# Moving the wait for a slot-table scatter from GpSimd to the load queue, the scatters behind the eighth sum, and an x2 copy ahead of a relu

## The reference

```python
for t in range(S):                        # attention, per batch and head: B, H, S, D = 4, 8, 768, 40
    m_new = np.maximum(f_gate[:, :, t] + m, i_gate[:, :, t])
    f_stab, i_stab = np.exp(f_gate[:, :, t] + m - m_new), np.exp(i_gate[:, :, t] - m_new)
    C = f_stab * C + i_stab * np.einsum('bhd,bhe->bhde', vt, kt)
    n = f_stab * n + i_stab * kt
    y[:, :, t] = sigmoid(o) * einsum(C, qt) / max(|n . qt|, 1)
x = y as (3072 tokens, 320)
h = x @ w_in                              # 320 x 2048
g = where(h >= 1, h, where(h <= -1, 0, (h + 1) ** 2 / 4))
x = g @ w_out                             # 2048 x 320
logits = x @ w_gate                       # 8 experts, the largest takes the token
out[mask] = gate_w * (relu(x[mask] @ w1[e]) @ w2[e])
```

## Time and profile before

| what | us |
|---|---|
| median of three runs | 878.41 (877.98 to 883.18) |
| the profiled execution, its own time | 891.37 |
| its span, first to last instruction | 889.5 |
| TensorE busy in the span | 792.6 (89%) |
| VectorE, ScalarE, GpSimd busy | 581.5, 407.9, 446.9 |
| mean granted TensorE clock, as a share of full speed | 0.958 |

### The profile page before, as it was taken

The page is one execution under the profiler, slowest core; times in us unless marked ns, Lnnn a source line. Parts: engine busy times, 40 slices in busy tenths (PEclk is TensorE's granted clock), DMA queues, the critical chain, the costliest instruction groups (busy, mean ns, idle before and its releaser), DMA issues.

```text
span 889.5 us, 17627 instructions
## 1 busy us (share of the span) xinstructions
PE 792.6 (89%) x5858; PEld 770.5 (87%) x5858; DVE 581.5 (65%) x965; ACT 407.9 (46%) x689; POOL 446.9 (50%) x357
## 2 busy tenths in 40 slices
PE   1799999899999999999899999806998999998975
PEld 1788999899989999999899999705998999998964
DVE  5565878597778877786878783445545666655440
ACT  2024454344444444453444444415656667666451
POOL 3352534344434434443443533326878887877742
PEclk9999999899999999999999999957999999999988
DMA  6931222424342332324222300040485313366730
GB/s 189 306 121 66 67 81 80 66 67 89 66 100 48 128 51 93 65 80 65 80 65 80 80 0 16 16 139 23 137 263 160 104 39 102 111 197 195 243 130 4
DMA packets 46887, 89.20 MB, mean 100 GB/s; under 512 B 6421, under 2 KB 29273, under 8 KB 46850
## 3 DMA queue, kind: packets, MB, share of 16 engines
q1 hardware_dynamic: 42962, 79.63, 32.4%
q0 software_dynamic: 3888, 9.08, 3.2%
HBM read 103.56 MB, written 9.33 MB: 127 GB/s over the span
## 4 chain that ended last, share of the span: by engine, by line
PE 54%; DMA 14%; issue 9%; DVE 8%; POOL 8%; ACT 4%; SPq 1%; POOLq 0%; DVEq 0%; ACTq 0%
PE bank L1270 14%; PE bank L1258 14%; DMA raw<-in_w 6%; PE bank L1449 6%; PE bank L1396 5%; DMA slot_table<-pair,dsti 4%; POOL w_tl L465 4%; PE bank L1214 3%; PE bank L1205 2%; PE bank L1230 2%; PE bank L1221 2%; POOL g_t L509 1%; PE bank L1411 1%; DVE g_l L951 1%; DMA tab<-slot_table,rowi 1%
## 5 line engine op out<-in xcount | busy, mean ns | idle before, releaser
L509 POOL TENSOR_TENSOR g_t<-u_t,r_t 128x512 f32<-128x512 f32 x96 | 132.3, 1378 | 216.6 <-ACT u_t L657 202.8
L652 ACT ACTIVATE r_t<-bank,neg 128x512 f32<-128x512 f32 x96 | 65.9, 686 | 220.2 <-PE bank L1258 195.9
L1270 PE MATMUL bank<-wo_h,g_h 128*128 128x328 f32 x384 | 130.1, 339 | 10.7 <-ACT x2s L669 8.7
L1270 PE MATMUL bank<-wo_h,g_l 128*128 128x328 f32 x384 | 122.8, 320 | 0.0
L1270 PE MATMUL bank<-wo_l,g_h 128*128 128x328 f32 x384 | 122.3, 319 | 0.0
L945 DVE TENSOR_SCALAR u_t<-bank 128x512 f32<-128x512 f32 x96 | 65.7, 685 | 78.1 <-ACT r_t L652 54.0
L1059 DVE TENSOR_TENSOR w_l<-raw,w_h 128x1024 fp32r<-128x1024 f32 x38 | 64.5, 1701 | 46.7 <-ACT w_th L723 46.5
L465 POOL TENSOR_TENSOR w_tl<-raw,w_th 128x512 fp32r<-128x512 f32 x38 | 72.5, 1931 | 30.9 <-ACT w_th L723 30.8
L1270 PEld LDWEIGHTS bank<-wo_h,g_h 128*128 128x128 f32 x384 | 74.5, 194 | 15.1 <-ACT x2s L669 10.1
L657 ACT ACTIVATE u_t<-u_t,half 128x512 f32<-128x512 f32 x96 | 69.4, 723 | 38.4 <-DVE u_t L945 38.4
L1258 PE MATMUL bank<-xT_h,wi_h 128*128 (+1 forms) x384 | 78.6, 287 | 1.6 <-issue 1.6
(11 more groups left out here) (210 smaller groups left out, 2084.0 us busy)
## 6 DMA issues: line engine op xcount, KB each, us to landing
raw<-in_w SPq DMA_DIRECT2D x19, 1280.0 KB
raw<-in_w SPq DMA_DIRECT2D x19, 1024.0 KB
W<-decays SPq DMA_DIRECT2D x24, 512.0 KB, 5.2
raw<-in_w SPq DMA_DIRECT2D x38, 256.0 KB
kS<-in_ktok SPq DMA_DIRECT2D x24, 256.0 KB
qT<-in_qt SPq DMA_DIRECT2D x48, 80.0 KB
kT<-in_kt SPq DMA_DIRECT2D x48, 80.0 KB
vS<-in_v SPq DMA_DIRECT2D x24, 160.0 KB, 5.1
```

The lines of the kernel that those rows point to most:

```text
L509: pool.tensor_tensor(g_t[p % 2][:, :], u_t[p % 2][:, :], r_t[p % 2][:, :], ALU.add).then_inc(sm["g_done"], 1)
L652: act.activation(r_t[p % 2][:, :], bank_h[p % 2][:, :], ACT.Relu, bias=neg1[:, 0:1]).then_inc(sm["r_done"], 1)
L1270: mm = pe.matmul(bank_acc[tt][:, 0:DL], l[p % 4][:, c], r[:, f, :], start=f == 0 and a == 0, stop=f == NT1 - 1 and a == 2)
```

## The change

The wait of `table_free` moves from GpSimd's program to the load queue's, behind `store_x2(t-1)`, with the first release of `pair`. GpSimd's `to_table` moves behind the sum of p = 7, and its waits for the last scatters stand ahead of the table's gather. ScalarE's `x2_copy` moves ahead of `relu_part(t, 2)`.

```diff
@@ block.sync
             for tt in range(2):
                 sp.sem_inc(x2_st[tt], 16)
+            sp.sem_inc(sm["pair_free"], 1)
@@ block.sync, behind store_x2
+            def table_free(t):
+
+                for tt in range(2):
+                    sp.wait_ge(slots_st[tt], (t + 1) * 16)
+                sp.sem_inc(sm["pair_free"], 1)
+
@@ block.sync, body
                 if prev:
                     store_x2(t - 1)
+                    table_free(t - 1)
@@ block.gpsimd
-            pool.sem_inc(sm["pair_free"], 1)
@@
-            def table_free(t):
-
-                for tt in range(2):
-                    pool.wait_ge(slots_st[tt], (t + 1) * 16)
-                pool.sem_inc(sm["pair_free"], 1)
-
@@ block.gpsimd, body and tail
-                    if prev and p == 7:
-                        to_table(t - 1)
                     gated(t, p)
                 if prev:
-                    table_free(t - 1)
+                    to_table(t - 1)
 
             def tail(t):
                 to_table(t)
-                table_free(t)
@@ block.gpsimd, behind all_blocks
+            for tt in range(2):
+                pool.wait_ge(slots_st[tt], 16 * NBLK)
             pool.wait_ge(sm["row_ready"], 1)
@@ block.scalar, body
                         x_high(t + 1, 0)
+                    if prev and p == 2:
+                        x2_copy(t - 1, 0)
+                        x2_copy(t - 1, 1)
                     relu_part(t, p)
@@
-                    if prev and p == 2:
-                        x2_copy(t - 1, 0)
-                        x2_copy(t - 1, 1)
                     square_part(t, p)
```

## The result

The changed kernel takes 983.34 us in the median of four runs (982.53 to 987.84), the kernel before 878.19 in the same session: a ratio of 1.117, 95% interval 1.112 to 1.121. That is 105.2 us more. The prediction was 975.0 us, with 948 to 1008 as its range. The profiled execution of the changed kernel took 982.53 us with a span of 980.7, so between the two profiled spans lie 91.2 us.

What follows compares the result with a forecast made beforehand. TensorE was taken to bound the stage. Nine bodies 11.1 us longer each add 99.6 us, the last block takes off 3.0, so 96.6 us on the median of 878.41 gives 975.0 us; range 948 to 1008.

Steps and rivals of the forecast that it cites:

- The mechanism: Load queue: next body's loads stand behind the wait for late scatters, so TensorE stalls ahead of L1205, nine times.
- The chain of the forecast: Block end at 406 us: last `first`, sum, scatters, landing, SP, kS load, then `scores`; a stall of 10.9 us.
- Half clock: TensorE returns from each stall at the lower clock level, 1.2 GHz, losing 1.7 us a block.
- The 3.3 us: Work TensorE does at half clock behind a stall, read from two earlier stretches; half of it is lost.
- the 40.83: TensorE's own work in one block, from the period 366.86 to 407.69 without idle stretches above half a microsecond.
- 53.4 us: New block period: 40.83 of work, 10.9 of stall, 1.7 of half clock; 11.1 us over 42.38.
- The DMA rule: Skill page's fixed cost of about 2.0 us for GpSimd-issued DMAs; each stall 2.1 us shorter, time about 956 us.
- The gain: TensorE's idle stretches and half clock in the old stage go: 1.55 us in each of nine periods.
- (a): Same stall but shorter: SP 0.2, kS 4.1, no clock lost, 3.1 us less in each of nine; 947 us, chance 0.18.
- (b): Longer stall: scatter lands in 6.5, kS only with W at 6.95, 4.35 us more each; 1014 us, chance 0.14.
- (c): The new wait is covered and the change only gains, 18 us less; 860 us, chance 0.03.
- (d): Stalls of 1 to 2 us that the gains pay, time within 1%; chance 0.03.

Runs made afterwards that it cites:

- e8: Changed kernel, but the load queue waits for block t-2's scatters ahead of the x2 store, and scatters are back ahead of the eighth sum: 865.56 us, ratio 0.981.
- e2: Changed kernel with scatters back ahead of the eighth sum and the x2 copy at its old place, leaving only the load queue's wait: 962.45 us, ratio 1.096.
- e9: e1 with both the x2 copy and the scatters at their old places: 867.70 us, ratio 0.970.
- e1: Changed kernel, but the load queue waits in body(t) for the scatters of block t-2, ahead of the x2 store: 871.53 us, ratio 0.991.
- e11: e8 timed once more, beside e9 on one chip: 865.72 us, ratio 0.967.
- e7: Changed kernel, but the next body's first-unit loads of qT, kT and kS are issued ahead of the wait for the scatters: 962.96 us, ratio 1.090.

## Why the prediction was right

**The mechanism** held step by step. The nine stalls sit ahead of L1205, released by kS. The chain of the forecast against the block end at 418: from the last matmul of the eighth `first` to the second scatter 5.5 us (forecast 5.95), landing 4.1 (4.1), SP 0.7 (0.7), qT's issue to `scores` 5.2 (5.1). The stall is 10.9 us in the mean of nine (10.9). The landing was 4.5 us in the mean, not 4.1, which made up for the shorter first part. That part is shorter because the scatter started 0.15 us behind the sum, not 0.81: in the last block of before VectorE's `dsti` was ready only at 568.03, as the sum ended, so the row timed the wait for `dsti` and not the issue alone.

**Half clock** was put too low, and the sum of the period hid it. TensorE's 5.3 us at 0.50 behind a stall lose half of that, 2.6 us, where I had 1.7. The periods say the same: 53.73 - 40.4 (e8's, without idle TensorE) - 10.9 = 2.4 us, and for e2 50.7 - 40.4 (e9's) - 7.8 = 2.5. The 3.3 us came from two stretches; the trace of before has a longer one at 171 us, behind 2.40 us of idle TensorE:

```profile
170.90:175.70 4.80, 4.78 (x19) 4.78 (x20) 4.13 (x10) 0.73 (x1) 1.32 (x2) 0.50 0.19 68
```

On the other side TensorE's own work is 40.4 us a block and not the 40.83 that I read from one period. The two errors point opposite ways, so that 53.4 us met 53.73 is in part luck. The stall of 10.9 us was measured by itself, with two of its terms 0.4 us off in opposite directions.

**The DMA rule** of the Trainium skill, page DMA: Bandwidth & Descriptors, section Anatomy of one DMA, puts at about 2.0 us the fixed cost of a DMA issued from GpSimd; the scatters took 3.0 to 6.3 here. With it the forecast would have been 956; the row was the better guide. **SP** waited 383.4 us on the scatters, some 35 us a time where I had written 25. I had counted from the old place of the loads, and the wait begins already behind the x2 store.

**The size that was off.** The time is 8.3 us above 975.0, and two terms make that up. Half clock is one: a stall and its half clock cost 13.3 us (53.73 - 40.4) and not 12.6, 6 us in nine. The gain is the other: "1.55 us in each of nine periods" and 3.0 in the last block, 17 us in all. It was right in size for the profiled execution that it was read from: e1's span is 18.0 us shorter. But I took it off the median of the timed runs with the words "the gap of 13 us between them I leave as it is". Against e8, whose TensorE has no idle time in the nine periods, before's median in e1's session is 13.3 us longer (878.87 to 865.56, two sessions), in e8's own 16.0, while the two profiled spans differ by 26.1 (889.5 to 863.4). So the timed runs held less of the losses than the profile, and the change took some 4 us less away than I subtracted. The timed runs have no trace, but their granted clock is on record: 0.965 in the median of the nineteen in e1's session, 0.958 in before's profiled execution, 0.969 in e8's and e1's runs. They had less half clock, as shorter waits would give. Together: 878.2, less the 13.3 us of gain, plus nine times the 13.3 us of stall and half clock, is 984.6 us, against the measured 983.34. e1's 7.3 us are no measure of this gain, since e1 is itself 6 us slower than e8, with a wait on xs that after does not have.

Between the two profiled spans the change is 91.2 us, and my 96.6 was 5 us too long there. The nine periods added 102.1 us where I had 99.6. Outside them the span fell by 10.9 us where I had 3.0. Part of that is the start, where before's first scatter at 153.08 is 2 to 3 us later than in its second profile (150.35) and in e8 (150.94); the rest was not followed up.

Rivals (a) and (b) asked for other landings and another clock than the trace shows; (c) and (d) for loads issued ahead of the scatters, which is what e1 is, and it gave 871.5 where (c) had 860 (865.6 in e8).

## What to carry to other kernels

A wait that is moved to a queue of loads has to be read with the indices of what stands behind it: here it was one block younger than the load behind it, and a prefetch made 20 us early turned into a chain of 15.5 us, 10.9 of them an idle TensorE. The same wait one block later in the same queue leaves no stall, and with the scatters left where they were it makes a kernel 1.9% faster than before in one session and 3.3% in another (e8, e11). Where a profiled execution lies far from the median of the runs, ask first whether the gap consists of the very waits that a change takes away; what is won then goes by the runs, not by the profile. And what half clock costs is best read behind every stall of a trace, not behind two: here they differ by a factor of nearly two.

## What the runs showed of the hardware

VectorE's scan (two inputs in SBUF) and GpSimd's sum did not run side by side: begun within 0.1 us of each other, the scan took 2.46 us, which is about its own 1.22 and the sum's 1.28; with the scan 0.34 us ahead, the sum took 1.97. The Trainium skill, page SBUF — State Buffer, section Who interferes with whom, says that a VectorE instruction with two SBUF inputs contends with a GpSimd instruction that reads SBUF; the traces agree. That this is the 6 us between e1 and e8 is the reading given above, and not tried apart.

Behind the nine stalls of after the granted clock stayed at 0.50 for 4.0 to 7.0 us of work, and behind those of e7 for 6.9 to 9.7.

The landing of two scatters of 1 KB varies. Beside the loads of a unit it took 9.0 us; in after, with no load in that time, it took 3.0 to 6.3, and two of the nine took over 6 us with no other transfer on the rings.
